# Reordering three instruction streams in the first phase of an FFT convolution and two split-precision MLP blocks: one filter load, one DVE subtraction, and six of the sixteen GpSimd weight residuals

## What is computed

```python
# x: (2, 3008, 256)
X = np.fft.rfft(x, axis=1)
y = np.fft.irfft(X * (filt_r + 1j * filt_i), n=3008, axis=1)     # 6016 tokens of 256
rms = np.sqrt(np.mean(y * y, axis=-1, keepdims=True) + 1e-06)
xn = y / rms * rms_g
g = xn @ w_gate                                                  # 256 -> 1536
z = (g / (1 + np.exp(-g)) * (xn @ w_val)) @ w_out                # 1536 -> 256
h = np.maximum(z @ w_in, 0.0)                                    # 256 -> 2048
out = (s * h * h + b) @ w_out2                                   # 2048 -> 256
```

## Time and profile before

| | |
|---|---|
| median of 3 runs | 1249.36 us |
| profiled execution, its own time | 1249.6 us |
| its span, first to last instruction | 1247.8 us |
| PE busy | 1240.2 us (99%) |
| DVE busy | 677.1 us (54%) |
| ACT busy | 554.7 us (44%) |
| POOL busy | 166.6 us (13%) |
| granted TensorE clock | 1.000 |

### The profile page before, as it was taken

The page is one execution under the profiler, slowest core; times in us unless marked ns, Lnnn a source line. Parts: engine busy times, 40 slices in busy tenths (PEclk is TensorE's granted clock), DMA queues, the critical chain, the costliest instruction groups (busy, mean ns, idle before and its releaser), DMA issues.

```text
span 1247.8 us, 20452 instructions
## 1 busy us (share of the span) xinstructions
PE 1240.2 (99%) x7268; PEld 1211.0 (97%) x7268; DVE 677.1 (54%) x1141; ACT 554.7 (44%) x1111; POOL 166.6 (13%) x167
## 2 busy tenths in 40 slices
PE   8999999999999999999999999999999999999998
PEld 5679999999999999999999999999999999999998
DVE  5677435454454444444444475555555555555555
ACT  3465433434243433343334365555555545555554
POOL 6575011101111011110120030000000000000000
PEclk9999999999999999999999999999999999999999
DMA  9863000000000000000010000000000000000000
GB/s 279 263 228 131 1 14 13 14 13 0 13 13 13 4 9 13 13 13 0 0 67 1 1 1 13 13 13 12 12 12 12 12 12 12 12 12 12 13 10 17
DMA packets 22519, 41.07 MB, mean 33 GB/s; under 512 B 1872, under 2 KB 18384, under 8 KB 21456
## 3 DMA queue, kind: packets, MB, share of 16 engines
q1 hardware_dynamic: 22480, 40.55, 10.1%
HBM read 28.10 MB, written 12.45 MB: 32 GB/s over the span
## 4 chain that ended last, share of the span: by engine, by line
PE 95%; POOL 2%; issue 2%; DMA 1%; DVE 0%; SPq 0%; ACT 0%; POOLq 0%
PE bank L388 30%; PE bank L389 30%; PE bank L390 30%; PE bank L373 2%; POOL spec L916 1%; PE bank L362 1%; DMA f<-filt 1%; PE bank L352 1%; PE bank L341 1%; PE bank L384 0%; PE bank L385 0%; POOL f L909 0%; POOL gate_lo L921 0%; POOL sq L931 0%; SPq L243 0%
## 5 line engine op out<-in xcount | busy, mean ns | idle before, releaser
L801 DVE TENSOR_TENSOR h<-bank,act 128x376 f32<-128x376 f32 x192 | 104.4, 544 | 309.1 <-PE bank L390 301.8
L832 DVE SCALAR_TENSOR_TENSOR h<-act,consts 128x376 f32<-128x376 f32 x256 | 159.6, 623 | 189.5 <-ACT act L667 185.5
L573 ACT ACTIVATE act<-bank 128x376 f32<-128x376 f32 x192 | 93.1, 485 | 357.4 <-PE bank L390 357.0
L667 ACT ACTIVATE act<-bank 128x376 f32<-128x376 f32 x256 | 124.1, 485 | 223.6 <-PE bank L390 223.6
L389 PE MATMUL bank<-h_lo,out_hi 128*128 128x376 f32 x512 | 171.4, 335 | 0.0
L390 PE MATMUL bank<-h_hi,out_lo 128*128 128x376 f32 x512 | 171.3, 335 | 0.0
L388 PE MATMUL bank<-xn_hi,in_hi 128*128 128x376 f32 x512 | 171.1, 334 | 0.2 <-issue 0.2
L388 PE MATMUL bank<-h_hi,out_hi 128*128 128x376 f32 x512 | 171.2, 334 | 0.0
L389 PE MATMUL bank<-xn_lo,in_hi 128*128 128x376 f32 x512 | 171.0, 334 | 0.0
L390 PE MATMUL bank<-xn_hi,in_lo 128*128 128x376 f32 x512 | 170.3, 333 | 0.0
L838 DVE SCALAR_TENSOR_TENSOR h_lo<-h,consts,h_hi 128x376 fp32r<-128x376 f32 x256 | 157.6, 616 | 0.2 <-ACT h_hi L676 0.2
(11 more groups left out here) (79 smaller groups left out, 2041.0 us busy)
## 6 DMA issues: line engine op xcount, KB each, us to landing
x_ring<-x SPq DMA_DIRECT2D x16, 384.0 KB, 7.3
f<-filt SPq DMA_DIRECT2D x8, 768.0 KB, 12.0
by_j<-w_b SPq DMA_DIRECT2D x4, 1536.0 KB, 6.7
z_ring<-by_j SPq DMA_DIRECT2D x32, 192.0 KB, 2.7
out<-staged SPq DMA_DIRECT2D x32, 188.0 KB, 1.9
in_raw<-w_in SPq DMA_DIRECT2D x1, 2048.0 KB, 7.7
out_raw<-w_out SPq DMA_DIRECT2D x1, 2048.0 KB, 7.7
gate_raw<-w_gate SPq DMA_DIRECT2D x2, 768.0 KB, 7.0
```

The source lines that it names most:

```text
L573: nc.scalar.activation(act[:, c % 2], bank[2 * (c % 2)][:, 0:TILE], ACT.Silu).then_inc(silu_done, 1)
L667: nc.scalar.activation(act[:, c % 2], bank[c % 4][:, 0:TILE], ACT.Relu).then_inc(relu_done, 1)
L801: nc.vector.tensor_tensor(h[:, c % 2], bank[2 * (c % 2) + 1][:, 0:TILE], act[:, c % 2], ALU.mult).then_inc(hmul_done, 1)
L832: nc.vector.scalar_tensor_tensor(out=h[:, c % 2], in0=act[:, c % 2], scalar=sc2, in1=act[:, c % 2], op0=ALU.mult, op1=ALU.mult).then_inc(q ...
```

## The change

Three lists are put in another order. No arithmetic, no tile, and no wait is changed.

```diff
@@ sync
             sp.dma_start(tabs[:, 0:TB2], tab[:, 0:TB2]).then_inc(tab1_in, 16)
             load_x(1)
+            load_f(0)
             sp.dma_start(tabs[:, TB2:], tab[:, TB2:]).then_inc(tab2_in, 16)
-            load_f(0)
             load_x(2)
@@ vector
             hmul(0, 0)
             hmul(0, 1)
+            low(0, 0)
             w1d_low(0)
-            low(0, 0)
@@ gpsimd, in the loop over q
                 elif q == 11:
-                    for i in range(2):
+                    for i in range(3):
                         w1_low(i)
                 elif q == 12:
                     squares(0)
                     square_sum(0)
                     square_split(0)
                 elif q == 13:
-                    for i in range(2, 6):
+                    for i in range(3, 6):
                         w1_low(i)
-                elif q >= 14:
-                    w1_low(2 * (q - 11))
-                    w1_low(2 * (q - 11) + 1)
+                elif q == 15:
+                    w1_low(6)
+                    w1_low(7)
@@ gpsimd, body
                 if is0(t):
-                    for i in range(10, PIECES1):
+                    for i in range(8, PIECES1):
                         w1_low(i)
                     gp.wait_ge(in2_in, 16)
```

## The result

| | kernel before | changed kernel |
|---|---|---|
| median of 4 runs | 1249.32 us | 1257.66 us |
| lowest to highest | 1249.07 to 1249.6 | 1256.34 to 1259.76 |
| ratio | | 1.0068, 95% interval 1.0051 to 1.0086 |
| profiled execution: time, span | 1249.6, 1247.8 | 1262.11, 1260.3 |
| mean granted TensorE clock | 1.000 | 0.995 |

The changed kernel is slower by 8.3 us, as forecast in sign (+4.3) and outside the range given (it ended at 1256.4). Its profiled execution is slower than all of its timed ones, by 2.4 us over the highest. So first its difference in span, 12.5 us, has to be taken apart, and then asked which of the parts the other executions had too. The four timed executions were 1257.88, 1256.34, 1257.45 and 1259.76 us, with mean granted clocks of 0.997, 1.000, 1.000 and 0.999.

What follows compares the result with a forecast made beforehand. TensorE (PE) was taken to bound the kernel, unbroken from 96 us on. GpSimd's edit +4.3 net, VectorE's 0 and SyncE's 0, on the median of 1249.4, gave 1253.7 us; range 1252.2 to 1256.4.

Steps and rivals of the forecast that it cites:

- What bounds the kernel: TensorE: busy 1240.2 of 1247.8 us, without a break from 96 us on, so any delay ahead is paid in full.
- +4.5: TensorE's start of gate_val(0,3), waiting for the tenth weight residual from GpSimd, moves from 96.0 to 100.5 us.
- VectorE's edit: Before down(0,0): w1d_low(0) behind low(0,0) costs 0.9 to 2.4 us by itself; value 0, hidden by GpSimd's edit.
- pieces 6 and 7: GpSimd, behind the totals of round 15: the pair takes 1.95 us, until 93.65, with VectorE waiting until 93.70.
- the squares: GpSimd's squares of tile 1, ahead of pieces 8 and 9: 4.50 us beside VectorE's low parts, until 98.15.
- pieces 8 and 9: GpSimd, behind the squares of tile 1, completing the count of 10: 2.3 us, the middle of 1.95 to 2.61.
- the faster normalisation: VectorE, with one GpSimd piece less in round 13: the last product of round 15 ends 0.54 us earlier, near 90.65.
- The -0.2 for the gap behind the stall: TensorE's 0.17 us gap ahead of down(0,1) at 98.40 vanishes when VectorE is far ahead: -0.2 us.
- rival (a): TensorE's clock falls from 2.4 to 1.2 GHz around the waits before down(0,0) and gate_val(0,3): 3.0 us more, 1256.7; chance 0.07.
- the value of 0: SyncE's filter tile 0 ahead of the second table piece gains TensorE nothing; ends -0.8 to +2.0 us.
- The same bytes lie ahead of tile 1 as before, so it doesn't move: At the start, sign(1) on GpSimd stays at 12.89 us, so TensorE's 1.26 us wait before step3(0,0) at 15.71 is unchanged.
- Rival (b): At the start, the tables land only with filter tile 1 and TensorE loses 2.0 us besides: 1255.7; chance 0.05.

Runs made afterwards that it cites:

- the fifteen stalls: Kernel before with six added reciprocals on VectorE ahead of low(t,3) in tiles 1 to 15: 1341.8 us, ratio 1.0723; stalls filled with matmuls: 1312.56, ratio 1.0487.

## Why the prediction was wrong, point by point

**What bounds the kernel.** Right. The part behind the third mark was 1138.6 us in every profile, and each microsecond lost ahead of it was paid in full (the kernels with the fifteen stalls set aside).

**GpSimd's edit: right mechanism, its term mis-sized.** The first step that failed is the sum "+4.5", from 91.19 to 100.5. It measured +5.29 with VectorE's edit and +5.50 without. POOL's rows in the changed kernel:

```profile
84.58 1.95 POOL L921 TENSOR_TENSOR val_lo<-val_raw,val_hi 128x384 fp32r<-128x384 f32 x2
89.17 1.00 POOL L916 TENSOR_TENSOR spec<-prod 128x384 f32<-128x384 f32 x1 [2.65 <-DVE prod L765]
...
96.20 1.01 POOL L916 TENSOR_TENSOR spec<-prod 128x384 f32<-128x384 f32 x1 [0.74 <-DVE prod L765]
97.16 2.00 POOL L921 TENSOR_TENSOR gate_lo<-gate_raw,gate_hi 128x384 fp32r<-128x384 f32 x2
99.09 1.76 POOL L931 TENSOR_TENSOR sq<-y 128x752 f32<-128x752 f32 x1
...
102.97 1.17 POOL L942 TENSOR_TENSOR ss_lo<-sq,ss_hi 128x376 fp32r<-128x376 f32 x1
104.10 1.93 POOL L921 TENSOR_TENSOR val_lo<-val_raw,val_hi 128x384 fp32r<-128x384 f32 x2
```

Item by item, with 4.77 taken off: pieces 6 and 7 took 2.00 us (forecast 1.95); the squares 5.01, from 99.09 to 104.10 (4.50), 0.32 of the excess in their first operation and 0.17 in their last, both started while a subtraction of DVE ran; pieces 8 and 9 1.93 (2.3); and the chain began 0.7 us late. That last one is the faster normalisation: it came, but its gain did not arrive. DVE's rows:

```profile
85.58 1.86 DVE L786 SCALAR_TENSOR_TENSOR y<-y,consts,rms 128x376 f32<-128x376 f32 x2
...
89.30 1.67 DVE L792 TENSOR_TENSOR xn_lo<-y,xn_hi 128x752 fp32r<-128x752 f32 x1 [0.21 <-ACT xn_hi L602]
...
99.49 1.79 DVE L775 TENSOR_TENSOR down_lo<-down_raw,down_hi 128x384 fp32r<-128x384 f32 x1
```

The pair took 1.86 instead of 2.60, as forecast (1.9). Then `total(14,0)` started at 89.17, and `xn_low`, at 89.30, took 1.67 us instead of the 0.94 of the earlier trace rows: what was left of the total, 0.87, and 0.80 for itself. Before, `xn_low` had started first, and the total paid for it. So the earlier one gains and the later one loses all of it. The Trainium skill ("SBUF — State Buffer", section "SBUF: two separate sides") gives this rule for a DVE operation with two SBUF inputs and a GpSimd operation that reads SBUF: whichever starts first has the shared port pair for the whole instruction. The trace agrees here to 0.15 us (0.87 and the 0.94 of its own are 1.81), and it was the rule, not the mean of two measured pairs, that should have gone into the sum; by it the forecast for the squares and for `xn_low` would have been dearer.

The -0.2 for the gap behind the stall was read off a row of PEld, the weight load, and not of PE. The third part did get shorter where the clock held, by 0.32 us (12.85 against 13.17), 0.20 of it at the start of `gate_val(0,3)`: the size is near by luck.

**The clock: a rival that should have been in the forecast.** Another step that failed is the weight of 0.07 on rival (a), with the argument that no fall was seen around 1.26 us of idle time and that `down(0,0)` splits the stall. It falls with the split stall in two of three profiles. Its size: 2.8, 1.5 and 0 us in the three profiles of the two kernels with both edits (third part less 12.85), 1.95 on average in the fifteen stalls of 3.8 us; I had 3.0. The Trainium skill ("TensorE: Matmul & The Clock Gate", section "What's actually happening") states that idleness throttles the array and activity releases it; the rows at 105 and 112 us agree. But in the timed executions of the result it can't be the main part of the miss: two of the four had a mean clock of 1.000.

**VectorE's edit.** Right: 2.27 us by itself (forecast 0.9 to 2.4), and hidden by GpSimd's: the stall part is 15.26 without it and 15.05 with it.

**SyncE's edit: the value of 0 failed, and the ratio of 0.9996 agrees with it by luck.** The step was "The same bytes lie ahead of tile 1 as before, so it doesn't move". It held in one profile of five, the one of that edit alone; in the others tile 1 was signed at 13.40 to 15.29 and `step3(0,0)` started at 16.22 to 18.51 instead of 15.71. Among executions with a mean clock of 1.000 the edit by itself costs 1.3 us (1250.78 against 1249.52). In the series of the experiments this was hidden by falls of the clock in the kernel before. In the result nothing hid it: its executions of the kernel before were all within 1249.07 to 1249.6. Rival (b), tables later than tile 0 by more than the slack, is seen in part in two profiles (12.22 and 10.56).

**The sum.** From 1249.3, 5.3 for the stall and -0.3 to +2.5 for the part behind it (12.85 to 15.63 against 13.17) give 1254.3 to 1257.1. The timed executions of the result are 1256.3 to 1259.8, and the two with a clock of 1.000 are 1256.34 and 1257.45, so 2.0 and 3.1 us over the sum without a fall. SyncE's edit with its 1.3 us brings that sum to 1255.6. The last 0.7 to 1.8 us in these two, and what makes 1259.76 at a clock of 0.999, are not shown: the start of a timed execution leaves no row. The forecast of 1253.7 missed the median by 4.0: 0.7 of it is the stall net of the gap, 1.3 the start as far as another series can tell, and the rest lies between the clock and late transfers and stays open.

## What to carry to other kernels

When a semaphore counts pieces, the place of the last piece needed is what matters. Before moving a piece, walk the list of the engine that makes it and add up all that now stands ahead, here 4.5 us of squares. When the bound engine comes to stand for some microseconds, ask for the price of its clock too: here 2 us for each stall of 3.8, and 0 to 2.8 behind stalls of 1.7 and 2.75. Compare executions of equal mean clock before calling an edit free: two effects may cancel in the medians. And where two engines share a port, find out who starts first in the new order instead of taking a mean duration.

## What the runs showed of the hardware that was not expected

- A stall of 2.75 us behind one of 1.7 let TensorE's clock fall to 0.50 in one execution of the same kernel and not in another (third ledger part 15.63 and 12.85). Fifteen stalls of 3.8 us cost 1.95 us each beyond the wait, at a mean clock of 0.973 in all four executions.
- A matmul on constants keeps the clock up: 3.3 us of them in each of the fifteen stalls made the kernel 29.2 us faster.
- One kernel's times split by its mean clock: 23 executions at 1.000 lie between 1248.65 and 1250.61, and 33 at 0.998 or lower between 1250.75 and 1255.84. Matmuls added to a gap of 1.3 to 1.6 us at 15 us made the second kind rare (2 of 24 against 13 of 34).
- Landing times at the start scatter between executions of one order: with the old one, filter tile 1 was signed at 12.50 to 13.04 us in five profiles and at 15.02 and 15.07 in two others, whose spectrum stage ended 4 to 5 us late. With the second table piece behind filter tile 0, the range was 12.93 to 15.29.
